# Second-layer rows turned by a crossbar DMA in 16-bit planes, and a reordered token split

## The chip, the cores and the metric

The kernel runs on one core of one Trainium2 chip. The metric is the device time of one execution in microseconds (us), as the median of the runs. An engine name in the rows is short: PE is TensorE, PEld its weight loads, DVE is VectorE, ACT is ScalarE, POOL is GpSimd, and SP is SyncE. SPq and ACTq are the DMA issues of SP and ACT.

## What is computed

Three stages follow each other. The change lies in the third (the second mixture of experts, called second layer here) and in the routing work that is done beside the middle one.

```python
def _moe_ref(x, w_gate, w_val, w_out):            # middle stage: 2304 tokens, 512 -> 1536 -> 512
    g = x @ w_gate
    return (g * (1 / (1 + np.exp(-g))) * (x @ w_val)) @ w_out

def _moe2_ref(x, w_gate, w_output_gate, w1, w2):  # last stage: 8 experts, 512 -> 1024 -> 512
    logits = x @ w_gate
    e_idx = np.argmax(logits, axis=1)
    ...                                           # gate_w: softmax value of the chosen expert
    eom = 1.0 / (1.0 + np.exp(-(x @ w_output_gate)))
    for e in range(E):
        mask = e_idx == e
        h = np.maximum(x[mask] @ w1[e], 0.0)
        out[mask] = gate_w[mask, None] * eom[mask, e, None] * (h @ w2[e])
```

## The kernel before

Every product is made of three float32 matmuls: each operand is split into a high part and a low part (what the high part leaves), and high*high, high*low and low*high are added in PSUM. So each matrix that goes into TensorE is first written twice, by ACT (high) and by DVE (low).

**Middle stage.** The loop over W goes through 4 blocks of 512 tokens; each block has 12 steps c. In a step PE makes the gate product and the value product (24 matmuls) and the output product of the step before (12 matmuls). Beside it, for W of 1 and more, the tokens of block W-1 are routed. On DVE this is `route(c)` (from L997): at c = 1, 2, 5 and 6 it splits a tile of y into three bf16 parts (`y_split_by_token`, L863 to L872, which waits for ACT's first part, `y_high`); at c = 4 and 8 it chooses the expert (`choose`); at c = 5 and 9 it finds each token's place (`place_tokens`) and writes one-hot matrices (`one_hots`, L921 to L925); at c = 6 and 10 it adds the result of PE to `places`. PE multiplies the one-hots in `place` (L1449) at the end of steps 5 and 9. SP turns the three bf16 parts with a DMA transpose (L413).

**Second layer.** The tokens are gathered by expert into tiles of 128 rows. Here there are 20 tiles: tiles 0 and 1 are written out by hand, tiles 2 to 19 run in a loop on each engine. For tile t PE does: `layer1` half 0 (12 matmuls of 512 columns, L1576), 6 matmuls of half 1, `turn_h(t, 0)` (4 transposes of the activations, L1591), the other 6 matmuls of half 1, `turn_rows(t+1)` (4 transposes of the next tile's rows out of `xg`, L1462), 3 matmuls of `layer2` (L1604), `turn_h(t, 1)`, and 21 more of `layer2`. Beside it:

- ACT: `relu(t, 0)` (L739), `h_high(t, 0)` (L734), `rows_high(t+1)` (L717, reads bank 2, into which PE turned the rows), `h_high(t, 1)`, `share(t)`.
- DVE: `h_low(t, 0)` (L1104), the relu of half 1 (L1241, signals `hb_ready`), `rows_low(t+1)` (L1099, signals `xt_ready`), `h_low(t, 1)`, `share(t)`, `scaled(t)` (L1113, needs `scale_in`, frees bank 7 by `o_ready`).
- POOL: waits for `xt_done` of tile t+1, gathers tile t+2 into `xg` by an indirect DMA (L559, L561), waits for the scatter of the tile before (`o_out`), copies the row numbers (L574, L575), looks the scales up by an indirect DMA (L533), and scatters the tile's result (L538) once `scaled(t)` is done.
- `share(t)` is this tile's share, if it has one, of splitting the next expert's weights: 4 chunks by ACT (`e_high`, L703) and DVE (`e_low`, L1095). SP loads the weights in bursts of 8 chunks of 512 KB (L424).

Each engine works through its instructions in the order of the program. Waits of PE in a tile: `ht_ready` (from `h_low(t, 0)`) ahead of layer2, `hb_ready` ahead of `turn_h(t, 1)`, `ht_ready` (from `h_low(t, 1)`) ahead of the 13th matmul of layer2, `o_ready` of the tile before ahead of layer2, and `xt_ready` ahead of layer1. `alone(engine, value)` puts a value into a register for a wait; it costs a register instruction.

Of the kernel before, what the change touches and what calls it, by code (L numbers as in the profile page):

```python
# [16 lines left out]
ALU = mybir.AluOpType  # L17
ACT = mybir.ActivationFunctionType
# [3 lines left out]
BF16 = mybir.dt.bfloat16  # L22
I32 = mybir.dt.int32
U32 = mybir.dt.uint32

P = 128


def build(nc, qT, kT, v, v_tail, w_phi, w_gate, w_val, w_out, w_router, w_outgate, w12, out):
# [4 lines left out]
    DM = H * D  # L34
# [41 lines left out]
    with ExitStack() as ctx:  # L76
        def sb(name, shape, dt=F32, scope=ctx):
            return scope.enter_context(nc.sbuf_tensor(name, shape, dt))
# [98 lines left out]
        h_sb = sb("h_sb", [P, EF])  # L177
        o_sb = sb("o_sb", [P, DM])
        row_in = sb("row_in", [P, 1], U32)
        row_out = sb("row_out", [P, 1], U32)  # L180
        place_rows = sb("place_rows", [P, PLACES], U32)
        scale_at = sb("scale_at", [P, PLACES], U32)
# [8 lines left out]
        t_i, t_per, t_rank, t_from, t_to, t1, t2, t3 = (sb(f"tt{i}", [P, SLOTS]) for i in range(8))  # L191
        n_used, n_tiles = (sb(n, [P, 1]) for n in ("n_used", "n_tiles"))
        eid_f, start_f = (sb(n, [P, E]) for n in ("eid_f", "start_f"))

        bank2 = [ctx.enter_context(nc.psum_tensor(f"bank{i}", [P, 2 * 512], F32)) for i in range(4)]
        bank = [bank2[i // 2][:, i % 2 * 512:(i % 2 + 1) * 512] for i in range(8)]
# [67 lines left out]
        second_in = sem("second_in")  # L264
        sc_in = sem("sc_in")
        xt_done = sem("xt_done")
        xthi_ready = sem("xthi_ready")
        xt_ready = sem("xt_ready")
        l1_done = sem("l1_done")
# [21 lines left out]
            return h_hi[:, c // 2, c % 2] if c < 4 else h_lo[:, c // 2 - 2, c % 2] if c < 8 else h_y[:, c - 8]  # L291

        TURNED = (NW - 1) * WT

        def both(x):

# [157 lines left out]
        def _(pool):  # L454
# [2 lines left out]
            pool.memset(ident[:], 0.0).then_inc(consts, 1)  # L457
            pool.memset(v_sb[:, :, :, D:V1, :], 1.0).then_inc(consts, 1)
            for i, (s, n) in enumerate(((lg_done, 1), (l2_done, 1), (o_ready, 1), (y_crossed, 32),
                         *((s, 16) for s in y_out))):  # L460
                pool.memset(credit[:, i:i + 1], 0.0).then_inc(s, n)
            pool.wait_ge(ones_ready, 1)
# [100 lines left out]

            pool.wait_ge(col_ready, 1)

            def gather_ahead(t):
                pool.wait_ge(xt_done, alone(pool, t + 2))
                gather(t + 2, pool.value_load(table[0:1, bass.ds(t + (T_COL + 2), 1)], min_val=0, max_val=PLACES - 1))

            def tile(t):  # L570
                gather_ahead(t)
                pool.wait_ge(o_out, alone(pool, t * 16))
                col = pool.value_load(table[0:1, bass.ds(t + T_COL, 1)], min_val=0, max_val=PLACES - 1)
                pool.tensor_copy(row_out[:], place_rows[:, bass.ds(col, 1)]).then_inc(ro_ready, 1)  # L574
                pool.tensor_copy(scale_row[:], scale_at[:, bass.ds(col, 1)]).then_inc(sr_ready, 1)  # L575
                pool.wait_ge(ro_ready, alone(pool, t - 1))
                pool.wait_ge(sr_ready, alone(pool, t - 1))
                scale_lookup(scale_rows, NT, scale_row[:, 0:1])
                scatter(t, row_out[:, 0:1])

            gather_ahead(0)
            gather_ahead(1)
            scatter(1, early_rows[:, 1:2])
            pool.wait_ge(tab_ready, 1)
            tiles = pool.value_load(table[0:1, T_TILES:T_TILES + 1], min_val=TILES, max_val=SLOTS)
# [2 lines left out]
            with pool.Fori(2, tiles) as t:  # L588
                tile(t)
            pool.wait_ge(xg_in, alone(pool, tiles * 16 + 16))  # L590
            pool.wait_ge(o_out, alone(pool, tiles * 16))

        @block.scalar
        def _(act):
# [142 lines left out]
            def relu(t, half):  # L737
                act.wait_ge(l1_done, t * 2 + (half + 1))
                act.activation(h_sb[:, half * 512:(half + 1) * 512], bank[half][:], ACT.Relu  # L739
                               ).then_inc(hb_ready if half else ha_ready, 1)  # L740

            def share(t):
                act.wait_ge(tab_ready, 2)
                h0 = act.value_load(table_w[0:1, bass.ds(t + W_FROM, 1)], min_val=0, max_val=2 * (E + 1))
                h1 = act.value_load(table_w[0:1, bass.ds(t + W_TO, 1)], min_val=0, max_val=2 * (E + 1))
                with act.If(h0 < h1):
                    with act.Fori(h0, h1) as half:
                        for i in range(HALF):
                            e_high(half, (half % 4) * HALF + i, i)
# [11 lines left out]
            store_scales(scale_rows, TILES, 2)  # L761
            h_high(1, 1)
            rows_high(2)
            share(1)

            tiles = act.value_load(table[0:1, T_TILES:T_TILES + 1], min_val=1, max_val=SLOTS)
            with act.Fori(2, tiles) as t:
                relu(t, 0)
                h_high(t, 0)
                rows_high(t + 1)  # L770
                h_high(t, 1)
                share(t)

        @block.vector
        def _(dve):
# [215 lines left out]
            def wide(W, first):  # L991
                def low(c):
                    dve.wait_ge(hi_ready, W * FC + (c + 1))
                    dve.tensor_tensor(both(h_lo[:, c % 2]), both(prod[:]), both(h_hi[:, c % 2]), ALU.subtract
                                      ).then_inc(lo_ready, 1)

                def route(c):  # L997
                    V = W - 1
                    for t, step in enumerate((1, 2, 5, 6)):
                        if c == step:  # L1000
                            y_split_by_token(V, t)
                    for i in range(2):
                        g, base = V * 2 + i, V * (2 * STEPS_R) + (i * STEPS_R + STEPS_0)
                        if c == 4 + 4 * i:
                            choose(g, base)
                        if c == 5 + 4 * i:
                            place_tokens(g, base)
                            one_hots(g)
                        if c == 6 + 4 * i:
                            add_places(g)  # L1010

                for c in range(FC):
                    if not first:
                        route(c)
                    dve.wait_ge(silu_done, W * FC + (c + 1))
                    if c or not first:
                        dve.wait_ge(lo_ready, W * FC + c)
                    dve.wait_ge(val_done, W * FC + (c + 1))
                    dve.tensor_tensor(both(prod[:]), both(silu[:]), bank[V_BANK][:], ALU.mult).then_inc(prod_ready, 1)  # L1019
                    low(c)  # L1020
# [196 lines left out]
                                         in1=t3[0:1, :], op0=ALU.min, op1=ALU.add).then_inc(tab_ready, 1)  # L1217


            def share(t):  # L1220
                dve.wait_ge(tab_ready, 2)
                h0 = dve.value_load(table_w[0:1, bass.ds(t + W_FROM, 1)], min_val=0, max_val=2 * (E + 1))
                h1 = dve.value_load(table_w[0:1, bass.ds(t + W_TO, 1)], min_val=0, max_val=2 * (E + 1))
                with dve.If(h0 < h1):
                    with dve.Fori(h0, h1) as half:
                        for i in range(HALF):
                            e_low(half, (half % 4) * HALF + i, i)
# [8 lines left out]

            tiles = dve.value_load(table[0:1, T_TILES:T_TILES + 1], min_val=TILES, max_val=SLOTS)
            with dve.Fori(2, tiles) as t:
                h_low(t, 0)
                dve.wait_ge(l1_done, t * 2 + 2)  # L1240
                dve.tensor_scalar(h_sb[:, 512:1024], bank[1][:], 0.0, None, ALU.max).then_inc(hb_ready, 1)  # L1241
                rows_low(t + 1)
                h_low(t, 1)
                share(t)
                scaled(t)

        @block.tensor
        def _(pe):
# [394 lines left out]
            with pe.Fori(2, tiles) as t:  # L1643
# [4 lines left out]
                layer1(t, rank, 1, 0, 2)  # L1648
                turn_h(t, 0)
                layer1(t, rank, 1, 2, KC)  # L1650
                turn_rows(t + 1)
                layer2(t, rank, 0, 1)
                turn_h(t, 1)
                layer2(t, rank, 1, EC)
# [45 lines left out]
```

## Time and profile before

| what | value |
|---|---|
| median of 3 runs (lowest, highest) | 885.0 us (882.47, 885.52) |
| the profiled execution's own time | 882.82 us |
| its span, first to last instruction | 881.1 us |
| busy share of PE, PEld, DVE, ACT, POOL | 97%, 81%, 44%, 29%, 19% |
| mean granted TensorE clock | 0.995 |
| share of PE in the chain that ended last | 87% |

The profile is one execution. The page lists busy time by engine and by group of instructions; the trace behind it can be asked for a stretch, a line or a tile. A row of a timeline gives start and length in us, the engine, the line of the kernel, the operation with output and inputs, how many were merged, and in brackets how long the engine had been idle before it and what ended that. Matmuls are pipelined, so a matmul of 0.39 us follows the one before after 0.23 us, and a weight load starts together with the matmul before its own.

### The profile page before, as it was taken

The page shows a single profiled execution, that of the slowest core. Times are in us where ns is not written, and L with a number is a line of the kernel's source. Part 1 is how long each engine was busy: PE and PEld are TensorE (multiplying, and loading weights), DVE is VectorE, ACT ScalarE, POOL GpSimd, SP SyncE. Part 2 cuts the span into 40 slices and gives each one's busy share as a digit, 9 for nine tenths or more (in the row PEclk, how much of TensorE's full clock was granted, in tenths as well). Part 3 has the DMA queues.
Part 4 walks back from the last instruction along what each step waited for, and adds up shares of the span by engine and source line. Part 5 has one row for each costly group of instructions (what it writes and reads, how often), then busy time and mean ns, then how long its engine had stood idle before and what let it go on. Part 6 is the DMA issues. An engine that isn't in the chain of part 4 may idle for free.

```text
span 881.1 us, 18909 instructions
## 1 busy us (share of the span) xinstructions
PE 850.6 (97%) x7048; PEld 713.7 (81%) x7049; DVE 385.9 (44%) x770; ACT 257.4 (29%) x387; POOL 163.2 (19%) x222
## 2 busy tenths in 40 slices
PE   8998998999999999999999999999989999999994
PEld 6888897888888788887888788998768888888883
DVE  5776896211132432324323432377774224534431
ACT  4564444111131112211132111325252213323311
POOL 5875300700000000000000000001022233323331
PEclk9999999999999999999999999999999999999997
DMA  9885743500011120203011010106511116116100
GB/s 265 256 240 163 222 139 110 155 0 1 1 61 24 20 65 0 65 18 83 0 48 36 18 42 0 49 2 230 214 49 42 41 48 226 42 39 229 41 25 18
DMA packets 70117, 73.26 MB, mean 83 GB/s; under 512 B 28590, under 2 KB 54830, under 8 KB 70064
## 3 DMA queue, kind: packets, MB, share of 16 engines
q1 hardware_dynamic: 63216, 49.92, 18.8%
q0 software_dynamic: 6560, 22.56, 8.1%
q8 instruction: 40, 0.66, 0.3%
q14 instruction: 13, 0.11, 0.0%
q10 hardware_dynamic: 288, 0.02, 0.0%
HBM read 54.11 MB, written 14.70 MB: 78 GB/s over the span
## 4 chain that ended last, share of the span: by engine, by line
PE 87%; DVE 3%; issue 3%; DMA 3%; ACT 1%; SPq 0%; POOL 0%; POOLq 0%; ACTq 0%; DVEq 0%
PE bank L1381 33%; PE bank L1400 14%; PE bank L1604 11%; PE bank L1576 11%; PE bank L1352 4%; PE bank L1270 4%; PE bank L1297 4%; PE bank L1591 2%; PE bank L1334 1%; PE bank L1462 1%; DMA e_w<-w 1%; PE bank L1371 1%; DMA k_sb<-kT 1%; PE bank L1422 1%; DMA y_rows<-y_sb 1%
## 5 line engine op out<-in xcount | busy, mean ns | idle before, releaser
L1019 DVE TENSOR_TENSOR prod<-silu,bank 128x512 f32<-128x512 f32 x48 | 32.9, 686 | 192.6 <-PE bank L1381 192.6
L1381 PE MATMUL bank<-x_hi,wg_hi 128*128 128x512 f32 (+1 forms) x240 | 90.9, 379 | 0.0
L1381 PE MATMUL bank<-x_hi,wg_lo 128*128 128x512 f32 (+1 forms) x240 | 88.4, 368 | 0.0
L1381 PE MATMUL bank<-x_lo,wg_hi 128*128 128x512 f32 (+1 forms) x240 | 88.3, 368 | 0.0
L1381 PE MATMUL bank<-x_hi,wv_hi 128*128 128x512 f32 (+1 forms) x240 | 88.3, 368 | 0.0
L1381 PE MATMUL bank<-x_lo,wv_hi 128*128 128x512 f32 (+1 forms) x240 | 88.3, 368 | 0.0
L1381 PE MATMUL bank<-x_hi,wv_lo 128*128 128x512 f32 (+1 forms) x240 | 88.3, 368 | 0.0
L528 POOL DMA_INDIRECT stage<-y_rows,early_rows x2 | 2.1, 1066 | 421.5 <-DVE early_rows L977 421.2
L660 ACT ACTIVATE silu<-bank 128x512 f32<-128x512 f32 x48 | 28.7, 598 | 168.3 <-PE bank L1381 168.3
L1400 PE MATMUL bank<-wo_hi,h_hi 128*128 128x512 f32 x192 | 75.5, 393 | 0.0
L1400 PE MATMUL bank<-wo_hi,h_lo 128*128 128x512 f32 x192 | 74.8, 390 | 0.0
L1400 PE MATMUL bank<-wo_lo,h_hi 128*128 128x512 f32 x192 | 74.7, 389 | 0.0
L654 ACT ACTIVATE h_hi<-prod 128x512 fp32r<-128x512 f32 x48 | 30.4, 632 | 150.5 <-DVE prod L1019 150.5
L1604 PE MATMUL bank<-e_hi,hT_hi 128*128 (+1 forms) x160 | 66.3, 414 | 1.5 <-issue 0.9
L1576 PE MATMUL bank<-e_hi,xgT_hi 128*128 (+1 forms) x160 | 64.4, 403 | 0.2 <-DVE xgT_lo L1099 0.2
L1604 PE MATMUL bank<-e_hi,hT_lo 128*128 (+1 forms) x160 | 62.6, 392 | 0.0
L1576 PE MATMUL bank<-e_hi,xgT_lo 128*128 (+1 forms) x160 | 62.6, 391 | 0.0
L1604 PE MATMUL bank<-e_lo,hT_hi 128*128 (+1 forms) x160 | 62.5, 390 | 0.0
L1576 PE MATMUL bank<-e_lo,xgT_hi 128*128 (+1 forms) x160 | 62.3, 390 | 0.0
L1104 DVE TENSOR_TENSOR hT_lo<-bank,hT_hi 128x512 fp32r<-128x512 f32 x40 | 27.7, 692 | 61.6 <-ACT hT_hi L734 60.5
L783 DVE TENSOR_REDUCE amax<-bank 128x8 f32<-128x1024 f32 (+1 forms) x40 | 44.6, 1115 | 20.4 <-PE bank L1270 20.2
L1381 PEld LDWEIGHTS bank<-x_lo,wv_hi 128*128 128x128 f32 x240 | 45.3, 189 | 7.5
(248 smaller groups left out, 1605.3 us busy)
## 6 DMA issues: line engine op xcount, KB each, us to landing
e_w<-w SPq DMA_DIRECT2D x32, 512.0 KB, 5.7
stage<-w_out POOLq DMA_DIRECT2D x16, 384.0 KB, 4.2
y_rows<-y_sb SPq DMA_DIRECT2D x18, 256.0 KB, 2.1
k_sb<-kT SPq DMA_DIRECT2D x16, 256.0 KB, 4.5
v_sb<-v SPq DMA_DIRECT2D x16, 256.0 KB, 4.8
q_sb<-qT SPq DMA_DIRECT2D x16, 256.0 KB, 3.6
x_rows<-x_sb SPq DMA_DIRECT2D x16, 256.0 KB, 3.9
x_in<-x_rows SPq DMA_DIRECT2D x4, 1024.0 KB, 5.7
```

The source lines that it names most:

```text
L654: act.activation(both(h_hi[:, c % 2]), both(prod[:]), ACT.Copy).then_inc(hi_ready, 1)
L660: act.activation(both(silu[:]), bank[G_BANK][:], ACT.Silu).then_inc(silu_done, 1)
L783: dve.tensor_reduce(top, proj, AX.X, ALU.max, apply_absolute_value=True).then_inc(amax_done, 1)
L1019: dve.tensor_tensor(both(prod[:]), both(silu[:]), bank[V_BANK][:], ALU.mult).then_inc(prod_ready, 1)
L1104: dve.tensor_tensor(hT_lo[:, at], bank[6 if half else 3][:], hT_hi[:, at], ALU.subtract).then_inc(ht_ready, 1)
L1270: mm = pe.matmul(acc, src[rows, h, j * P:min((j + 1) * P, S)], phi[rows, :], start=True, stop=True)
L1297: mm = pe.matmul(sums(c, i)[cols, :], feat[:, s, sign, at:at + TAIL], v_sb[:, j, 2 * c + hh, :, a], start=(j == 0 and i in (0, 7)), stop=F ...
L1352: mm = pe.matmul(acc, feat[:, s, sign, half * 512 + i * TAIL:half * 512 + (i + 1) * TAIL], kv_sb[:, b, h // 2 if j < JF else half, sign * ...
L1381: mm = pe.matmul(acc[:, 0:width], w[:, k, cols], x[:, k, 0:width], start=(k == 0 and i == 0), stop=(k == KC - 1 and i == 2))
L1400: mm = pe.matmul(bank[O_BANK + t][:], h[:, c % 2, t // TT, cols], w[:, c, :], start=(c == 0 and i == 0), stop=(c == FC - 1 and i == 2))
L1576: mm = pe.matmul(bank[half][:], x[:, at], w_part(w, rank, k * EF + half * 512), start=(k == 0 and i == 0), stop=(k == KC - 1 and i == 2))
L1604: mm = pe.matmul(bank[7][:], h[:, at], w_part(w, rank, HALF_W + k * DM), start=(k == 0 and i == 0), stop=(k == EC - 1 and i == 2))
```

## The change

Tiles 3 and later of the second layer are no longer turned by PE. The float32 rows are read as pairs of 16-bit words. POOL copies the two words into two planes (`part_words`), ACT issues one DMA transpose of both planes (`cross`), DVE joins the turned planes into `xT` (`merge`), and the high and low parts are made from `xT` in SBUF in place of bank 2 (`merged_high`, `merged_low`). Gathers run three tiles ahead in place of two; tile 3 goes into the second buffer. In the middle stage `y_split_by_token` moves behind `place_tokens`, `one_hots` and `add_places` of the same step.

```diff
             for i, (s, n) in enumerate(((lg_done, 1), (l2_done, 1), (o_ready, 1), (y_crossed, 32),
+                         (x_crossed, 16), (x_merged, 2),
@@ POOL
-            def gather_ahead(t):
-                pool.wait_ge(xt_done, alone(pool, t + 2))
-                gather(t + 2, pool.value_load(table[0:1, bass.ds(t + (T_COL + 2), 1)], min_val=0, max_val=PLACES - 1))
+            def part_words(slot):
+                for half in range(2):
+                    pool.tensor_copy(planes[:, half, :], words(xg_second if slot else xg)[:, :, half]).then_inc(planes_ready, 1)
             def tile(t):
-                gather_ahead(t)
+                pool.wait_ge(xg_in, alone(pool, t * 16 + 16))
+                pool.wait_ge(x_crossed, alone(pool, t * 16))
+                part_words(0)
+                pool.wait_ge(planes_ready, alone(pool, t * 2))
+                gather(t + 3, pool.value_load(table[0:1, bass.ds(t + (T_COL + 3), 1)], min_val=0, max_val=PLACES - 1))
                 pool.wait_ge(o_out, alone(pool, t * 16))
...
-            gather_ahead(0)
-            gather_ahead(1)
+            pool.wait_ge(xt_done, 1)
+            gather(2, column(2))
+            pool.wait_ge(xt_done, 2)
+            pool.tensor_copy(row_second[:], place_rows[:, bass.ds(column(3), 1)]).then_inc(ri_ready, 1)
+            pool.wait_ge(ri_ready, 2)
+            pool.indirect_dma_start(xg_second, None, y_rows, bass.IndirectOffsetOnAxis(ap=row_second[:, 0:1], axis=0),
+                                    bounds_check=NT - 1, oob_is_err=False).then_inc(second_in, 16)
+            pool.wait_ge(xt_done, 3)
+            gather(4, column(4))
+            pool.wait_ge(second_in, 32)
+            part_words(1)
             scatter(1, early_rows[:, 1:2])
@@ ACT
+            def cross(u, n):
+                act.wait_ge(planes_ready, alone(act, n * 2))
+                act.wait_ge(x_merged, alone(act, n * 2))
+                act.wait_ge(consts, 6)
+                act.dma_start_transpose(planesT[:].rearrange("p a (c n) -> p (a c) n", n=P),
+                                        planes[:].rearrange("p a d -> p (a d)")).then_inc(x_crossed, 16)
+            def merged_high(t):
+                act.wait_ge(l1_done, t * 2 + 2)
+                act.wait_ge(x_merged, alone(act, t * 2))
+                act.activation(xgT_hi[:], xT[:], ACT.Copy).then_inc(xthi_ready, 1)
             rows_high(2)
+            cross(3, 1)
             share(1)
             with act.Fori(2, tiles) as t:
                 relu(t, 0)
                 h_high(t, 0)
-                rows_high(t + 1)
+                merged_high(t)
                 h_high(t, 1)
+                cross(t + 2, t)
                 share(t)
@@ DVE
                 def route(c):
-                    for t, step in enumerate((1, 2, 5, 6)):
-                        if c == step:
-                            y_split_by_token(V, t)
                     for i in range(2):
                         ...                       # choose, place_tokens, one_hots, add_places
+                    for t, step in enumerate((1, 2, 5, 6)):
+                        if c == step:
+                            y_split_by_token(V, t)
+            def merge(t):
+                dve.wait_ge(x_crossed, alone(dve, t * 16))
+                for half in range(2):
+                    dve.tensor_copy(words(xT[:])[:, :, half], planesT[:, half, :]).then_inc(x_merged, 1)
+            def merged_low(t):
+                dve.wait_ge(xthi_ready, t + 2)
+                dve.tensor_tensor(xgT_lo[:], xT[:], xgT_hi[:], ALU.subtract).then_inc(xt_ready, 1)
             with dve.Fori(2, tiles) as t:
+                merge(t)
                 h_low(t, 0)
                 ...                               # relu of half 1
-                rows_low(t + 1)
+                merged_low(t)
@@ PE
                 layer1(t, rank, 1, 2, KC)
-                turn_rows(t + 1)
                 layer2(t, rank, 0, 1)
```

## Rows read from the trace of the kernel before

**Rows 1.** Windows: one tile each; busy us by engine (instructions), clock, DMA share, GB/s.

```profile
645.39:659.78 14.39, 13.06 (x61) 10.40 (x62) 9.81 (x13) 9.19 (x12) 4.72 (x7) 1.00 0.19 56
...
728.64:740.92 12.28, 12.28 (x62) 10.19 (x61) 3.52 (x6) 2.39 (x4) 3.59 (x6) 1.00 0.52 161
```

**Rows 2.** Timeline of a tile: start us, us, engine, line, operation, [idle before <-releaser].

```profile
738.63 0.69 DVE L1104 TENSOR_TENSOR hT_lo<-bank,hT_hi 128x512 fp32r<-128x512 f32 x1 [3.85 <-ACT hT_hi L734]
...
738.96 0.39 PE L1576 MATMUL bank<-e_hi,xgT_lo 128*128 x1
...
739.19 0.60 PE L1462 MATMUL bank<-ident,stage 128*128 128x128 f32 x4
739.39 0.69 DVE L1241 TENSOR_SCALAR h_sb<-bank 128x512 f32<-128x512 f32 x1
...
740.09 0.40 PE L1604 MATMUL bank<-e_hi,hT_lo 128*128 x1
740.13 0.55 PEld L1591 LDWEIGHTS bank<-ident,h_sb 128*128 128x128 f32 x4
```

**Rows 3.** Timeline, the last step-5 value and output products and place, W of 1.

```profile
296.99 0.39 PE L1400 MATMUL bank<-wo_hi,h_lo 128*128 128x512 f32 x1
...
297.49 0.35 DVE L925 TENSOR_SCALAR hot_col<-iota_f,g_col,token_no 128x144 fp32r<-128x144 f32 x1
...
298.18 0.44 PE L1381 MATMUL bank<-x_hi,wg_hi 128*128 128x512 f32 x1
```

**Rows 4.** Timeline, the same place in step 9 of the same W.

```profile
331.71 0.40 PE L1400 MATMUL bank<-wo_hi,h_lo 128*128 128x512 f32 x1
...
332.13 0.44 PE L1381 MATMUL bank<-x_hi,wg_hi 128*128 128x512 f32 x1
```

**Rows 5.** Timeline, the engines beside PE from tile 1's end into tile 2.

```profile
645.65 1.05 POOL L561 DMA_INDIRECT stage<-y_rows,row_in  x1 [0.85 <-POOL row_in L559]
646.17 3.90 ACT L703 ACTIVATE e_hi<-e_w  x4 [1.72 <-issue]
...
652.77 0.68 DVE L1104 TENSOR_TENSOR hT_lo<-bank,hT_hi 128x512 fp32r<-128x512 f32 x1
```

**Rows 6.** Tile view of y_tok: durations ns min/median/max, first and last start; time to landing.

```profile
L870 DVE CAST y_tok<-y_sb x12: 427/427/428, 260.4 to 509.4; 128x512 bf16<-128x512 f32 x12
...
L413 SPq DMA_TRANSPOSE y_parts<-y_tok x12: 1280/1430/1543, 261.7 to 513.3; - x12
...
DMA to landing us min/median/max: 3.6/3.7/3.8
```

**Rows 7.** Groups of POOL by line and shape: count, busy us, mean ns, idle before.

```profile
L524 POOL TENSOR_TENSOR wo_lo<-stage,wo_hi 128x768 fp32r<-128x768 f32 x8 | 14.8, 1845 | 48.3 <-DMA x_rows<-x_sb 45.2 <-DMA stage<-w_out 3.0
...
L517 POOL CAST wo_hi<-stage 128x768 fp32r<-128x768 f32 x8 | 6.7, 832 | 4.8 <-DMA stage<-w_out 4.8
...
L559 POOL COPY row_in<-place_rows 128x1 uint32 x20 | 3.7, 186 | 58.3 <-PE bank L1462 56.8 <-issue 1.5
```

**Rows 8.** Timeline, first share tile of the loop and the tile under a weight load.

```profile
656.77 3.91 ACT L703 ACTIVATE e_hi<-e_w  x4 [1.14 <-issue]
...
664.97 0.69 DVE L1104 TENSOR_TENSOR hT_lo<-bank,hT_hi 128x512 fp32r<-128x512 f32 x1 [1.54 <-ACT hT_hi L734]
...
743.96 1.26 POOL L574 COPY row_out<-place_rows 128x1 uint32 x1 [1.17 <-DMA out<-o_sb,row_out]
...
750.91 0.69 DVE L1104 TENSOR_TENSOR hT_lo<-bank,hT_hi 128x512 fp32r<-128x512 f32 x1 [0.49 <-ACT hT_hi L734]
```

**Rows 9.** Timeline, the scales' lookup, PE's last matmul and the scatter of the last tile.

```profile
866.75 1.02 POOL L533 DMA_INDIRECT scale_in<-scale_rows,scale_row  x1 [0.87 <-POOL scale_row L575]
868.10 0.39 PE L1604 MATMUL bank<-e_hi,hT_lo 128*128 x1
868.91 0.75 DVE L1113 TENSOR_SCALAR o_sb<-bank,scale_in 128x512 f32<-128x512 f32 x1 [3.85 <-DMA scale_in<-scale_rows,scale_row]
870.55 1.02 POOL L538 DMA_INDIRECT out<-o_sb,row_out  x1 [2.78 <-DVE o_sb L1113]
```

More of the change, by code:

```diff
@@ L24 @@
 U32 = mybir.dt.uint32
+U16 = mybir.dt.uint16
 P = 128
@@ L179, in build @@
         row_in = sb("row_in", [P, 1], U32)
+        row_second = sb("row_second", [P, 1], U32)
         row_out = sb("row_out", [P, 1], U32)
@@ L193, in build @@
         eid_f, start_f = (sb(n, [P, E]) for n in ("eid_f", "start_f"))
+        planes, planesT = (sb(n, [P, 2, DM], U16) for n in ("planes", "planesT"))
+        xT = sb("xT", [P, KC * P])
         bank2 = [ctx.enter_context(nc.psum_tensor(f"bank{i}", [P, 2 * 512], F32)) for i in range(4)]
@@ L266, in build @@
         xt_done = sem("xt_done")
+        planes_ready = sem("planes_ready")
+        x_crossed = sem("x_crossed")
+        x_merged = sem("x_merged")
         xthi_ready = sem("xthi_ready")
@@ L293, in build, with words @@
         TURNED = (NW - 1) * WT
+        def words(x):
+            return x.bitcast(U16).rearrange("p (n w) -> p n w", w=2)
         def both(x):
@@ L564, in _, with column @@
             pool.wait_ge(col_ready, 1)
-            def gather_ahead(t):
-                pool.wait_ge(xt_done, alone(pool, t + 2))
-                gather(t + 2, pool.value_load(table[0:1, bass.ds(t + (T_COL + 2), 1)], min_val=0, max_val=PLACES - 1))
-            def tile(t):
-                gather_ahead(t)
+            def column(u):
+                return pool.value_load(table[0:1, bass.ds(u + T_COL, 1)], min_val=0, max_val=PLACES - 1)
+            def part_words(slot):
+                for half in range(2):
+                    pool.tensor_copy(planes[:, half, :], words(xg_second if slot else xg)[:, :, half]).then_inc(planes_ready, 1)
+            def tile(t):
+                pool.wait_ge(xg_in, alone(pool, t * 16 + 16))
[3 more added lines that the diff above has]
+                gather(t + 3, pool.value_load(table[0:1, bass.ds(t + (T_COL + 3), 1)], min_val=0, max_val=PLACES - 1))
                 pool.wait_ge(o_out, alone(pool, t * 16))
@@ L590, in _ @@
             pool.wait_ge(xg_in, alone(pool, tiles * 16 + 16))
+            pool.wait_ge(x_crossed, alone(pool, tiles * 16))
             pool.wait_ge(o_out, alone(pool, tiles * 16))
```

## The prediction

> **What bounds the kernel now.** I read the page's part 1 first: PE is busy for 97% of the span, as the table of the section on the profile has it. A busy matmul record overlaps its neighbour, so this share hides short waits. I therefore went on to windows of one tile of the second layer, and then to timelines of the places that the change touches. A tile of the loop takes 12.28 us in which PE shows no gap, while DVE is busy for 3.5 us and ACT for 2.4 us, at a granted clock of 1.00 [rows 1]. Only tile 2, the first of the loop, is longer: 14.39 us. So what counts is PE's order of work, and for each piece taken out of it, what PE must wait for just behind that piece.
>
> **Removed: turn_rows, 18 times.** The reader should look at three starts in [rows 2]. The last matmul of layer1 starts at 738.96 and the third of layer2 at 740.09. That is 1.13 us, and three steps between matmuls are 3 x 0.23 = 0.68 us (738.96 to 739.19 is one step). So turn_rows costs PE 0.45 us, and 18 of them are 8.1 us. Then I ask what is late next. Behind turn_rows come three matmuls and `turn_h(t, 1)`, which needs DVE's relu of half 1. That relu needs the last matmul of layer1 (738.96 + 0.39 = 739.35), starts at 739.39, lasts 0.69 and so ends at 740.08. The weight load of `turn_h(t, 1)` starts at 740.13, where the matmul ahead of it would have let it start at 740.09 [rows 2]. The turn sits exactly at the end of the relu already. Without turn_rows PE would be there at 739.64 and wait until 740.13. The high part is no help either: the first matmul of layer2 needs `h_low(t, 0)`, which runs from 738.63 to 739.32, while PE would now arrive at 739.19. Nothing after the relu becomes shorter. **The period of a plain tile stays at 12.28 us; turn_rows was free.** I put 0 on this term, with 0.04 us on either side for 17 tiles, so -0.7 to +0.7.
>
> **Moved: one-hots ahead of the split.** In step 5 of each W of 1 to 3, DVE splits a tile of y and only then writes the one-hots; the last one-hot starts at 297.49 and PE, whose last output matmul started at 296.99, comes to the next gate product at 298.18 [rows 3]. In step 9, where nothing is split, the same distance is 332.13 - 331.71 = 0.42 us [rows 4]. So the wait costs 1.19 - 0.42 = 0.77 us, three times, 2.3 us. The trace has the same idle time in all three W. With the new order the one-hots start as soon as PE has counted the tokens, before the gate product of the step; the split still waits for ACT's part, as before, so its DMA transpose leaves when it did. **-2.3 us**, and I see nothing that takes its place.
>
> **Added ahead of tile 2: ACT waits for POOL.** `cross(3, 1)` stands ahead of `share(1)` and `relu(2, 0)` on ACT. It needs both planes of tile 3, and POOL makes these only after it issued the gather of tile 4. That issue is the one at 645.65 now, ending at 646.70 [rows 5]. What a plane copy costs on POOL no row shows. The nearest is a cast of 768 elements in 832 ns, so 512 take 0.55 us; the bounds are the 0.19 us of a copy of one element and the two-input operation at 1845 x 512/768 = 1.23 us [rows 7]. I take 0.55, since a copy has one input. The planes are ready at 646.70 + 1.1 + 0.1 = 647.9. The issue of a DMA transpose holds a queue for 1.43 us at 384 KB [rows 6]; for 256 KB I take two thirds, 0.95 us (bounds 0.3 and 1.54). Then `share` needs its register loads and branch, the 1.0 to 1.1 us of idle time marked "issue" [rows 8]. So the weight split starts at about 649.9 in place of 646.17 [rows 5]: 3.7 us later. DVE's four `e_low` follow, then `scaled(1)`, and `h_low(2, 0)` at 652.77 with no idle time before it; PE waits for that one. New on this path are also the two join copies: 0.43 us each by the DVE cast of 512 elements [rows 6], 0.69 as upper bound (`h_low` in [rows 2]), 0.2 as lower. Total 3.7 + 0.9 = **+4.6 us**, once, bounds +2.7 and +7.7. PE has nothing to do meanwhile. The gather of tile 3 goes out ahead of that of tile 4 in time that POOL spent waiting.
>
> **Added to tiles with a share: 5 in the loop.** ACT now issues the crossing between `h_high(t, 1)` and the weight split (+0.95), and DVE joins between `scaled` and `h_low(t+1, 0)` (+0.9). The idle time ahead of that `h_low` is 1.54 us in three such tiles and 0.49 us in the two that run under a weight load, where `scaled` is held by the scales' landing and not by the split [rows 8]. The first kind loses 0.95 + 0.9 - 1.54 = 0.3 us, the second 0.9 - 0.49, with a little for the split, 0.6 us. 3 x 0.3 + 2 x 0.6 = **+2.2 us**, bounds 0 and +5.5.
>
> **Hidden in plain tiles.** The crossing leaves ACT about 4 us before the tile's end, and lands 3.7 us after its issue, by the transposes of y [rows 6]; the join is wanted from DVE 1.3 us after the tile's start, and may be 3 us late before it delays `h_low`. Making `merged_high` and `merged_low` from SBUF is the same count of operations. POOL's new copies fill time in which it waited for `xt_done`.
>
> **The end.** The last `scaled` waits for the scales (866.75 issued, 868.91 used [rows 9]), and PE's last matmul ends at 868.10 + 0.39 = 868.49. POOL no longer waits for turn_rows and issues the lookup 1 to 2 us earlier: **-0.4 us**, bounds -0.5 and 0.
>
> **The sum.** 0 - 2.3 + 4.6 + 2.2 - 0.4 = +4.1 us. On the profiled execution's 882.8 us (span 881.1) this is 886.9. The median is 885.0, 2.2 above it, so I forecast 889.1, rounded to **889.0 us**.
>
> **A rule weighed against the rows.** During a weight split on DVE a POOL copy of one element lasts 1.26 us, as in [rows 8], against the 0.19 of such a copy in [rows 7]. The Trainium skill, "SBUF — State Buffer", section "Who interferes with whom", says why: a DVE instruction with two SBUF inputs and a GpSimd instruction that reads SBUF exclude each other for a whole instruction. The trace agrees. If POOL's plane copies fell into the split of a share tile, the rule would add about 1.1 us to DVE in each of 5 tiles; by POOL's order they come after the scatter, which comes after the split, so my sum goes without it.
>
> **The rivals.**
> (a) PE's gain arrives. If `turn_h(t, 1)` were not bound by the relu, 17 tiles would give 7.7 us: 889.0 - 7.7 = 881.3. Against it stands the start at 740.13 [rows 2], 0.05 us behind the relu.
> (b) The wait ahead of tile 2 is not there, or hidden: 889.0 - 4.6 = 884.4. For it: I infer POOL's and ACT's order from the code, and the issue may be quick. Against it: ACT is in order, and PE waited for the same chain before. With (a) too it would be 876.7.
> (c) Slower: POOL becomes the bound. Its cycle is a closed chain: two plane copies; 0.1; row copy 0.2 after 0.9 of loads; gather 0.85 + 1.05 [rows 5]; two small copies 0.3; lookup 0.87 + 1.02, then 1.14 until `scaled`, then 1.64 until the scatter, 1.02 [rows 9]. Together 9.1 us and the two copies. It decides from (12.28 - 9.1)/2 = 1.6 us a copy. At 1.85 us (the longest POOL operation of [rows 7]) each tile takes 12.8 us, and 17 tiles add about 9 us: 898. A crossing that lands more than 3 us later than those of y, as two do perhaps under a weight load, acts at the same place, DVE's join ahead of `h_low`.
>
> **How the numbers follow.** Forecast 0.50, for 885 to 894 by the bounds of its terms taken together; (b) alone 0.15; (a) alone 0.13; (a) with (b) 0.05; (c) 0.17. About 0.5% (4.4 us) is what a measurement of this kernel can tell from no change. Faster, below 880.6: (a) with (b), and 0.06 of each of (a) and (b), 0.17. Slower, above 889.4: (c) and 0.24 of the forecast, 0.41. Within: 0.42. The range is 880 to 898, which leaves out (a) with (b) and the upper part of (c).
>
> **What would show it.** Plain tiles at 12.28 us with PE idle for about 0.4 us ahead of L1604 or `turn_h(t, 1)`, released by DVE, confirm the first step; 11.8 us refutes it. Tile 2 of about 19 us, with ACT idle ahead of `e_high` until POOL's planes, confirms the third. A plane copy over 1.6 us, or DVE idle ahead of the join for a DMA in plain tiles, means (c). Step 5 without the 0.77 us confirms the second. The prediction is wrong if the join or the plane copies are far from 0.43 and 0.55 us, or if the issue on ACT doesn't hold its queue.

## The result and the profile after

The changed kernel takes 908.15 us (median of 4 runs, 903.62 to 912.19) against 884.24 us before; the ratio is 1.027, interval 1.0215 to 1.0326. That is 24 us slower. I had forecast 889 us and a range up to 898, so the sign was right and the size was not: the time lies outside the range. The profiled execution is the slowest of the four.

The page of the profiled execution (912.19 us, span 910.1), part 1:

```profile
span 910.1 us, 18958 instructions
...
PE 855.8 (94%) x6976; PEld 712.8 (78%) x6977; DVE 399.0 (44%) x806; ACT 257.9 (28%) x387; POOL 184.3 (20%) x264
```

PE has 72 instructions less and a busy share of 94% in place of 97%: it waits more. To see where, I compare the distance between two tiles, from one `turn_h(t, 1)` to the next, read from PE's timeline (the starts of its second group of four transposes in each tile; tile 9, for example, goes from 739.47 to 751.66).

```
us from turn_h(t-1,1) to turn_h(t,1)   t=2    3      4-9    10     11     12-14  15     16     17-19
before                                 16.99  12.27  12.28  12.28  12.28  12.28  12.28  12.28  12.28
changed kernel                         23.44  13.57  12.20  19.06  13.53  12.23  20.49  14.04  12.22
```

The plain tiles are 0.05 to 0.08 us shorter and the time is lost in six tiles: tile 2 (+6.5), tile 3 (+1.3), tiles 10 and 11 (+8.0) and tiles 15 and 16 (+10.0). Together with the plain tiles' -0.8 that is 25 us. The routing of the middle stage gives back 2.3 us. From the place of step 5 (the product with the one-hots) to that of the next block it is 103.13 us before and 102.35 us after, twice, and the first of these places comes 0.71 us sooner after the stage's first gate product. Together this is 22.7 us, which meets the 24 us of the medians within a microsecond or two. In this one execution the span also holds 5.8 us more ahead of the middle stage, in the attention stage, whose code is the same; the first gate product starts anywhere from 147.6 to 156.7 us in the profiled executions of this study, so I count that to none of the parts.

Tile 8's end of the changed kernel, the rows that answer to [rows 2] (a timeline, columns as there):

```profile
737.84 0.69 DVE L1149 TENSOR_TENSOR hT_lo<-bank,hT_hi 128x512 fp32r<-128x512 f32 x1 [3.45 <-ACT hT_hi L764]
...
738.61 0.69 DVE L1297 TENSOR_SCALAR h_sb<-bank 128x512 f32<-128x512 f32 x1
738.67 0.49 PE L1660 MATMUL bank<-e_hi,hT_hi 128*128 x1
...
739.35 0.26 PEld L1647 LDWEIGHTS bank<-ident,h_sb 128*128 128x128 f32 x2 [0.16 <-DVE h_sb L1297]
```

The first matmul of layer2 now comes 0.14 us after `h_low` ended (738.53), and the weight load of `turn_h(t, 1)` 0.05 us after the relu ended (739.30). PE waits twice where the four transposes stood.

The first of the slow tiles, 2, on ACT, DVE and POOL, answering to [rows 5]:

```profile
650.66 1.17 POOL L584 COPY planes<-stage 128x512 uint16<-128x512 uint16 x2
...
652.06 1.35 ACTq L777 DMA_TRANSPOSE planesT<-planes  x1
655.81 3.90 ACT L733 ACTIVATE e_hi<-e_w  x4 [7.41 <-issue]
659.61 0.57 ACT L769 ACTIVATE h_sb<-bank 128x512 f32<-128x512 f32 x1
...
662.40 0.79 DVE L1269 COPY xT<-planesT 128x512 uint16<-128x512 uint16 x2
663.07 0.68 DVE L1149 TENSOR_TENSOR hT_lo<-bank,hT_hi 128x512 fp32r<-128x512 f32 x1
```

ACT sat idle for 7.41 us ahead of `e_high`, first for the planes and then for its own issue, and the relu of tile 2 stands behind the split. PE shows the same as a wait of 6.53 us ahead of `turn_h(2, 0)`; it then runs at a granted clock of 0.50 until 664 us, which stretches the three matmuls ahead of `turn_h(2, 1)` by 0.2 us.

And tile 10, which no term of my sum has. Timeline of the changed kernel again:

```profile
752.45 1.37 ACTq L777 DMA_TRANSPOSE planesT<-planes  x1
...
756.28 1.02 POOL L545 DMA_INDIRECT scale_in<-scale_rows,scale_row  x1 [0.87 <-POOL scale_row L595]
...
767.12 0.75 DVE L1158 TENSOR_SCALAR o_sb<-bank,scale_in 128x512 f32<-128x512 f32 x1 [5.60 <-DMA scale_in<-scale_rows,scale_row]
767.78 0.78 DVE L1269 COPY xT<-planesT 128x512 uint16<-128x512 uint16 x2
768.46 0.68 DVE L1149 TENSOR_TENSOR hT_lo<-bank,hT_hi 128x512 fp32r<-128x512 f32 x1
...
769.28 0.79 PE L1660 MATMUL bank<-e_hi,hT_hi 128*128 x1 [6.32 <-DVE hT_lo L1149]
```

The lookup of 128 scales is issued at 756.28 and used at 767.12; such a lookup lands in 2.6 us at the median. The crossing issued at 752.45 lands after 13.7 us, where the median of all 19 is 3.4. DVE waits 5.60 us for the scales, so `scaled`, the join and `h_low` all come late, and PE waits 6.32 us. The tile view of `planesT` has the spread of the crossings:

```profile
L1269 DVE COPY xT<-planesT x36: 442/450/457, 662.4 to 886.6; 128x512 uint16<-128x512 uint16 x36
L777 ACTq DMA_TRANSPOSE planesT<-planes x19: 1249/1254/1371, 652.1 to 892.9; - x19
...
DMA to landing us min/median/max: 3.1/3.4/14.2
```

What else is in flight is seen in windows of 2 us of both kernels (us, granted clock, DMA share, GB/s). An expert's weights are loaded from 733.98 us before and from 745.39 us after. Before:

```profile
741.00:743.00 2.00, 1.00 1.03 422
743.00:745.00 2.00, 1.00 1.02 414
745.00:747.00 2.00, 1.00 1.00 381
747.00:749.00 2.00, 1.00 0.67 270
749.00:751.00 2.00, 1.00 0.01 0
```

After:

```profile
754.00:756.00 2.00, 1.00 1.02 418
756.00:758.00 2.00, 1.00 1.33 284
758.00:760.00 2.00, 1.00 1.17 119
760.00:762.00 2.00, 1.00 0.97 186
762.00:764.00 2.00, 1.00 0.42 146
764.00:766.00 2.00, 1.00 0.31 112
766.00:768.00 2.00, 0.68 0.01 4
768.00:770.00 2.00, 0.50 0.00 0
```

Before, the load keeps about 400 GB/s until it is done, 15 us after its start. After, the rate is still 418 GB/s in the window ahead of 756 us and 119 from 758 us, some 5 us after the crossing was issued, and the load ends 21 us after its start. The crossing, the lookup and the load's last chunk all land between 766.1 and 767.1 us; the gather issued at 750.98 lands after 9.7 us, where the others take 2.7 to 3.9. The last two windows show a second, small loss: while PE waits, from 763 us on, the granted clock goes to 0.50, the lower of its two levels (1.2 GHz). The stretch from the first matmul of layer2 to `turn_h(10, 1)` then takes 1.54 us (769.28 to 770.82), where tile 8 has 0.80.

### The profile page after: what moved, and what is told of

Read it like the earlier page. It is cut to its first block, busy times and chain, and to the rows that moved or that the text cites. A ratio compares the mean times of both kernels' runs of the same rounds, so it can differ in the third digit from the quotient of the medians.

```text
span 910.1 us, 18958 instructions
## 1 busy us (share of the span) xinstructions
PE 855.8 (94%) x6976; PEld 712.8 (78%) x6977; DVE 399.0 (44%) x806; ACT 257.9 (28%) x387; POOL 184.3 (20%) x264
## 3 DMA queue, kind: packets, MB, share of 16 engines
q10 hardware_dynamic: 20352, 5.00, 3.4%
## 4 chain that ended last, share of the span: by engine, by line
PE 82%; DMA 7%; issue 4%; DVE 3%; ACTq 1%; POOL 1%; ACT 1%; POOLq 0%; SPq 0%; DVEq 0%
PE bank L1437 32%; PE bank L1456 14%; PE bank L1660 10%; PE bank L1632 7%; PE bank L1408 4%; PE bank L1326 4%; PE bank L1353 4%; DMA scale_in<-scale_rows,scale_row 3%; DMA out<-o_sb,row_out 2%; PE bank L1647 1%; PE bank L1390 1%; PE bank L1427 1%; DMA e_w<-w 1%; DMA k_sb<-kT 1%; PE bank L1478 1%
## 5 line engine op out<-in xcount | busy, mean ns | idle before, releaser
L1660 PE MATMUL bank<-e_hi,hT_hi 128*128 (+1 forms) x160 | 68.7, 429 | 17.8 <-DVE hT_lo L1149 16.0
L1660 PEld LDWEIGHTS bank<-e_hi,hT_hi 128*128 128x128 f32 x160 | 31.1, 194 | 31.8 <-issue 25.6
L1437 PEld LDWEIGHTS bank<-x_hi,wg_lo 128*128 128x128 f32 x240 | 45.2, 188 | 7.6
```

The source lines that it names most:

```text
L1437: mm = pe.matmul(acc[:, 0:width], w[:, k, cols], x[:, k, 0:width], start=(k == 0 and i == 0), stop=(k == KC - 1 and i == 2))
L1660: mm = pe.matmul(bank[7][:], h[:, at], w_part(w, rank, HALF_W + k * DM), start=(k == 0 and i == 0), stop=(k == EC - 1 and i == 2))
```

## The experiments

Two theories stood against each other for tiles 10 and 15. A: a crossing and a weight load in flight together slow each other and all that lands then. B: the crossing as such is harmless, and the new order of POOL's work, or the new chain of waits, puts something late. Tile 2 had its own theory, the queue of ACT.

**e1_order: the first part of the change alone, on the kernel before.**

```diff
                 def route(c):
-                    for t, step in enumerate((1, 2, 5, 6)): ...  # y_split_by_token
                     for i in range(2): ...                       # choose, place, one_hots, add_places
+                    for t, step in enumerate((1, 2, 5, 6)): ...  # y_split_by_token
```

> The kernel before with one part of the change alone: in the routing of the middle stage the token split of a step stands behind the one-hots. The theory of the prediction: PE's wait of 0.77 us at the end of step 5 goes in each of three blocks, nothing takes its place, -2.3 us (ratio 0.9974); the distance from the place of step 5 to that of the next block falls from 103.13 to 102.36 us. Rival: the split now stands between the one-hots and the product of its own step, and another wait takes over, ratio 1.000 or above. In the changed kernel the distance is 102.35 us, but its start of the second layer is 4 us later than before, so this run also says whether that shift belongs to this part of the change (then the first gate product, at 149.99 us before and 155.83 us in the changed kernel, comes late here too) or not.

Measured: 879.86 us against 884.16, ratio 0.9958 (0.9937 to 0.9978). From the place of step 5 to that of the next block it is 102.35 us (296.84 to 399.19), as in the changed kernel. In step 5 the last one-hot and PE's use of it stand far apart now:

```profile
291.33 0.35 DVE L925 TENSOR_SCALAR hot_col<-iota_f,g_col,token_no 128x144 fp32r<-128x144 f32 x1
292.79 0.69 DVE L868 TENSOR_TENSOR y_sb<-y_sb,y_tok 128x512 f32<-128x512 f32 x1 [1.11 <-issue]
...
296.61 0.42 PEld L1449 LDWEIGHTS bank<-hot_col,hot_row 128*128 128x128 f32 x2
```

So the part gives 2.3 us by the trace; the ratio says 1.9 to 5.6 us. Its attention stage is not late (first gate product at 149.61), which speaks against this part as the source of the 5.8 us there. All tiles of the second layer take 12.28 us and tile 2 16.98.

**e2_cross_late: the first crossing behind the first weight split.**

```diff
-            cross(3, 1)
             share(1)
+            cross(3, 1)
```

> The changed kernel with one line moved: ACT issues the first crossing behind the first weight split in place of ahead of it. Theory: tile 2 was late because ACT waited for POOL's planes and then for the issue, with the weight split and the relu queued behind. Then the distance from turn_h(1, 1) to turn_h(2, 1), 23.44 us in the changed kernel and 16.99 before, falls to about 18.5 (the relu waits only for the issue of about 1.4 us, and the join for the crossing's landing), some 5 us in all, ratio about 0.022 above before in place of 0.027. Rival: the wait only moves to the join, because the crossing leaves 3 us later than it could, and tile 2 stays above 22 us. Tiles 10, 11, 15 and 16 should stay as late as in the changed kernel by either.

Measured: 900.49 us, ratio 1.018 (1.0139 to 1.0221). Tile 2 takes 17.82 us in place of 23.44, 5.6 us less, and 0.8 more than before. ACT's timeline:

```profile
646.13 2.01 ACT L733 ACTIVATE e_hi<-e_w  x2 [1.78 <-issue]
646.60 1.17 POOL L584 COPY planes<-stage 128x512 uint16<-128x512 uint16 x2
648.00 1.36 ACTq L777 DMA_TRANSPOSE planesT<-planes  x1
648.04 1.99 ACT L733 ACTIVATE e_hi<-e_w  x2
```

The split starts 1.78 us after the row work, as in [rows 5], and ACT's sequencer issues the crossing while its datapath still works off the split. So the loss of tile 2 was the place in ACT's queue. The rival, that the join would wait instead, is out. Tiles 10 and 15 stay at 18.11 and 20.31 us.

**e3_plain_copy: the crossing as a plain copy.** Tiles 3 and later are computed from rows that are not turned.

```diff
-                act.dma_start_transpose(planesT[:].rearrange("p a (c n) -> p (a c) n", n=P),
-                                        planes[:].rearrange("p a d -> p (a d)")).then_inc(x_crossed, 16)
+                act.dma_start(planesT[:].rearrange("p a d -> p (a d)"),
+                              planes[:].rearrange("p a d -> p (a d)")).then_inc(x_crossed, 16)
```

> The changed kernel in which the crossing is a plain DMA of the same 256 KB on the same queue with the same waits; the rows of tiles 3 and later are left unturned, so the result of those tiles is not the reference's. Theory A: the transpose itself, with its many small packets, collapses the DMA rate when it is in flight with a weight load (tiles 10 and 15 of 19.06 and 20.49 us for 12.2). Then a plain copy lands in 3 to 5 us beside the load, those tiles fall to 12.2 to 13.5 us, and the kernel takes about 893 us (ratio 1.010). Theory B: any transfer whose landing DVE needs in that place is as late, and the scales' lookup, which POOL now issues in the midst of the load, is late by itself: then tiles 10 and 15 stay at 19 to 20 us and the ratio at 1.027. The lookup of tile 10 took 10.8 us to land in the changed kernel, 2.4 us in its place before.

Measured: 887.41 us, ratio 1.0039 (1.0014 to 1.0064), less than the 1.010 that theory A had. Tiles 10 and 15 take 12.85 and 12.88 us, tiles 11 and 16 12.69 and 12.72, tile 3 12.23. POOL's order, the waits and the bytes are those of the changed kernel, so theory B falls for this place. The lookups under the load still take 4.9 us to land here, both times, and the gathers 6.3 and 7.2; in the changed kernel it was 10.8 and 12.2, and 9.7 and 8.2. So a load by itself slows them too, but far less. Tile 2 stays at 22.93 us, which agrees with e2: a wait for POOL, not for a landing. Windows of this kernel under a load (busy by engine, then clock, DMA share, GB/s as above), and its issue on ACT from the tile view of `planesT`:

```profile
754.00:756.00 2.00, 2.00 (x10) 1.65 (x9) 1.16 (x2) 2.00 (x3) 0.77 (x3) 1.00 1.04 422
756.00:758.00 2.00, 2.00 (x10) 1.68 (x9) 2.00 (x3) 1.38 (x2) 0.97 (x1) 1.00 1.03 412
```

```profile
L777 ACTq DMA_DIRECT2D planesT<-planes x19: 480/481/537, 652.7 to 875.8; - x19
```

**e7_idle_cross: the crossing by itself, beside the kernel before.** `planes` is set to zero once by POOL; nobody reads `planesT`; the only waits on it are ACT's own, ahead of the next crossing and at the end.

```diff
                 rows_high(t + 1)
                 h_high(t, 1)
+                cross(t)
                 share(t)
```

> The kernel before, with one more DMA transpose of 256 KB of 16-bit zeros per tile, issued by ACT at the place where the change issues its crossing; nothing in the kernel uses it, PE still turns the rows, POOL's order is that of before. This measures the crossing by itself. Theory A (a crossing in flight with a weight load slows both, and all that lands at that time): the crossings of the tiles under a load land after 8 to 14 us in place of 3.4, the scales' lookup and the gather beside them land late, and tiles 10 and 15 take several us more although nobody waits for the crossing: ratio 1.006 to 1.018. Theory B (the order of POOL's work puts the lookup into the load): lookups stay at 2 to 3 us, and only the queue time on ACT shows: the weight split starts 2 us later and share tiles take up to 0.8 us more, ratio 1.000 to 1.004.

Measured: 903.43 us, ratio 1.0221 (1.0184 to 1.0258), more than I had given theory A. Tiles 10 and 15 take 21.32 and 19.89 us, tiles 11 and 16 13.78 and 14.38, tile 2 18.28; tiles without load or split 12.28. Windows of 2 us, and what waited in tile 10:

```profile
744.00:746.00 2.00, 1.00 1.03 418
746.00:748.00 2.00, 1.00 1.36 358
748.00:750.00 2.00, 1.00 1.18 124
750.00:752.00 2.00, 1.00 1.23 101
```

```profile
748.32 1.02 POOL L537 DMA_INDIRECT scale_in<-scale_rows,scale_row  x1 [0.87 <-POOL scale_row L580]
...
761.25 0.75 DVE L1127 TENSOR_SCALAR o_sb<-bank,scale_in 128x512 f32<-128x512 f32 x1 [7.85 <-DMA scale_in<-scale_rows,scale_row]
```

```profile
760.34 1.11 PE L1476 MATMUL bank<-ident,stage 128*128 128x128 f32 x4 [6.18 <-DMA stage<-y_rows,row_in]
```

The crossing was issued at 743.65. No engine is held up by it, yet the lookup that is in flight with it lands after 12.9 us (median 2.3), and PE waits 6.18 us for the rows of the gather issued at 744.45. In the tiles without a load the lookups land in 2.2 to 2.5 us, though a crossing leaves some 3 us ahead of them, so it takes the load too. This run alone shows a loss nearly as large as that of the change, though PE meets it at another wait: for the gathered rows, which the changed kernel fetches a tile earlier.

Tile 2's 1.3 us are not of the crossing, since the first one leaves behind `turn_h(2, 1)` (656.79). The only new work ahead of it is POOL's clearing of `planes` at the end of tile 1, which I take for the cause, though no run leaves it out:

```profile
639.82 0.97 POOL L569 MEMSET planes<- 128x1024 uint16 x1
...
657.59 1.36 ACTq L760 DMA_TRANSPOSE planesT<-planes  x1
```

**e5_split_load: the crossing and the load kept apart in time.** On the changed kernel, SP waits ahead of the fifth of the eight chunks.

```diff
                 for c in range(CH):
+                    if c == HALF:
+                        sp.wait_ge(x_crossed, alone(sp, start * 16 + 16))
                     load_chunk(e, j, c)
```

> The changed kernel with one wait added: SP issues the second four chunks of an expert's weight load only when the crossing of that tile has landed, so a crossing and a load are never in flight together; the bytes, the transposes and POOL's order stay. Theory A (the crossing and the load slow each other when together): every crossing lands in 3 to 4 us, the lookups in 2.3 to 4 us, tiles 10 and 15 (19.06 and 20.49 us in the changed kernel) fall to about 13 us, tiles 11 and 16 stay near 13.5 for the weight split, and some 15 us go: ratio 1.010 (1.005 to 1.014). Theory B (only the wait structure and POOL's order matter): tiles 10 and 15 stay above 17 us. A third way: the second half of the load comes too late for its split and ACT waits for the chunks, then tile 11 and 16 go above 15 us.

Measured: 890.13 us, ratio 1.0078 (1.004 to 1.0115), as theory A had it. Tiles 10, 11, 15 and 16 take 12.88, 13.65, 13.06 and 13.64 us; tile 2 stays at 23.97. The same transposes and the same bytes, one wait more, and 17 us less by the ratios, 13.3 us by the tiles of the loop: theory A. The crossing (745.25) still meets the last of the load's first half, whose traffic ends at 749 us, without such a loss.

**e8_idle_split and e9_idle_split_same_tile: the idle crossing with the load split.**

```diff
+                    if c == HALF:
+                        sp.wait_ge(x_crossed, alone(sp, start * 16 + 32))    # e8; + 16 in e9
```

> The kernel before with the idle crossing of the run e7_idle_cross (which took 1.0221 of the time of before), and the second half of each weight load held until the tile's crossing has landed. Theory A: the idle crossing costs only where it meets the load; kept apart, tiles 10 and 15 fall from 21.32 and 19.89 us to about 12.3 to 13, and what is left is tile 2 (+1.3) and the hold of ACT's queue in tiles with a split (0 to 1 us each): ratio 1.003 (1.000 to 1.007). Theory B (the crossing costs wherever it is issued, for example by what follows it on ACT): the ratio stays above 1.015.

e8 measured 900.82 us, ratio 1.0194 (1.0163 to 1.0225). That was far from the expected 1.003, and the ratio says nothing on the theories, since my count was wrong by one crossing: the second half of a load waited for the next tile's crossing, ACT waited for its chunks, and tiles 11 and 16 took 20.66 and 19.24 us. Tiles 10 and 15, where the crossing now met at most half a load, took 12.50 and 12.27.

> As e8_idle_split, with the count of the wait mended: there the second half of the load waited for the crossing of the next tile, came a tile late, and tiles 11 and 16 took 20.66 and 19.24 us for the chunks. Now it waits for the crossing of its own tile. Theory A (the crossing costs only where it meets the load): tiles 10, 11, 15 and 16 take 12.3 to 13 us, and the ratio is 1.003 (1.000 to 1.007). Theory B (the crossing costs more wherever it is issued): above 1.010.

e9 measured 887.54 us, ratio 1.006 (1.0028 to 1.0092), in place of the 1.0221 of e7. Tiles 10 and 15 take 13.93 and 13.49 us, somewhat more than expected, tiles 11 and 16 12.35 and 12.33, tile 2 18.24. Against e7 this is 14 us by the ratios and 17 us by the tiles: so much the crossing costs where it meets the load. The 4.4 us by which the loop is still longer than before are something else. Tile 2 has the same 1.3 us as in e7, and in tiles 10 and 15 `scaled` waits 1.46 and 1.13 us for the scales, whose lookup meets the second half of the load and lands after 6.5 and 6.2 us:

```profile
753.65 0.75 DVE L1129 TENSOR_SCALAR o_sb<-bank,scale_in 128x512 f32<-128x512 f32 x1 [1.46 <-DMA scale_in<-scale_rows,scale_row]
```

**e6_all and e10_share_first: towards a version without the losses.** e6 joins e2 and e5; e10 also issues the loop's crossing behind the weight split.

```diff
                 h_high(t, 1)
-                cross(t + 2, t)
                 share(t)
+                cross(t + 2, t)
```

> The changed kernel with both cures: the first crossing behind the first weight split, and the weight load in two halves around the crossing. By the terms measured so far against the kernel before: one-hots -2.3 us (ratio 0.9958 as measured alone), plain tiles -0.07 us each or -0.8, tile 2 +0.8, four or five tiles with a split +1.3 each or +5 to +6: about +3 us, ratio 1.003 (0.999 to 1.008). If the crossing has a cost that lies neither in the collision nor in ACT's queue, it is above 1.010. It is not expected to beat the one-hots part alone (0.9958).

e6 measured 888.10 us, ratio 1.0061 (1.0038 to 1.0083).

> The kernel e6_all (ratio 1.0061) with one more line moved: in the loop ACT makes its weight split first and issues the crossing behind it, so the split no longer stands behind the crossing's issue. Theory: tiles with a split (3, 10, 11, 15, 16: 12.9 to 13.65 us in e6_all) lose their 0.7 to 1.4 us because the split starts 2.3 us late behind the crossing; here they come to 12.2 to 12.6 us, about 4.5 us in all, ratio 1.001 (0.998 to 1.004). Rival: the crossing, leaving 5 us later in those tiles, lands after the join should have run, and the same 1 us is lost there (ratio unchanged); by the landing of 3.4 us and the 4.3 us that the join can wait, this should just not happen.

e10 measured 882.33 us, ratio 0.9991 (0.9959 to 1.0024). Tile 3 goes from 13.62 us in e6 to 12.49 and tile 15 from 12.91 to 12.22, as the theory has it; tile 16 hardly moves (13.60 to 13.55), and tile 10 gets worse (12.94 to 14.90). In both, DVE now waits for the scales (2.36 and 3.07 us): POOL's two copies of one element ahead of the lookup run beside the split and last up to 1.2 us each, against 0.2 elsewhere, and the join stands behind `scaled`. With all three cures the loop still takes 5.0 us more than before (230.68 against 225.70 us from `turn_h(1, 1)` to `turn_h(19, 1)`), in an execution of 887.27 us, 5 above its kernel's median; the one-hots give 2.3 back, and the medians show no difference. e1 (0.9958) is the fastest kernel here by the median; its interval and that of e10 overlap.

## Why the prediction was wrong

**turn_rows: right.** I said that removing it gives nothing since the relu of half 1 and `turn_h(t, 1)` come next. The plain tiles went from 12.28 to 12.20 to 12.23 us, 12 of them by 0.07 us on average: -0.8 us, against 8.1 us of removed work. The two waits of PE stand where I put them.

**One-hots: right.** -2.3 us forecast; measured 354.18 us before and 351.90 after from the first gate product to the third place of step 5, -2.3 us, and 0.9958 alone.

**Tile 2: right mechanism, size too small.** Forecast +4.6 us (bounds 2.7 to 7.7), measured 23.44 - 16.99 = +6.5. The plane copies came out at 1.17 us for two (I had 1.1), and the joins put `h_low` 0.67 us later (0.9). The issue on ACT lasted 1.35 us (0.95), and what I had as 1.0 us of register loads behind it took 2.4 us: 652.06 + 1.35 = 653.41, and the split starts at 655.81. The plain copy of e3 has nearly the same 2.2 us behind an issue of only 0.54. A DMA issue doesn't only hold the queue: it looks as if the register loads, which ACT otherwise does while it still computes (1.0 to 1.1 us are left of them in [rows 8]), start after it. No row shows these loads by themselves. The rest is the lower clock, 0.2 us.

**Share tiles: right mechanism, size too small.** Forecast +2.2 us for five (bounds 0 to 5.5). With the collision out of the way (e5), tiles 3, 10, 11, 15 and 16 take 13.56, 12.88, 13.65, 13.06 and 13.64 us, that is +5.4 us. It is the same term: ACT starts the split 2.8 to 3.6 us after `h_high` ended, where it was 1.0 to 1.1, and DVE goes from the split through `scaled` and the join to `h_low` without a pause. e10 takes this away in tiles 3 and 15; in tiles 10 and 16 the scales then hold the same chain.

**The end: nothing.** From `turn_h(19, 1)` to the end of the span it is 18.0 us in both. `scaled` starts 0.67 us after PE's last matmul began, in place of 0.81. The 0.4 us that I had taken are the time from PE's end to DVE's start, of which 0.3 us stay though the scales no longer hold it.

**The step that failed: "a crossing that lands more than 3 us later than those of y, as two do perhaps under a weight load".** I had put this as half a sentence into rival (c), with no price of its own, and priced (c) as a POOL cycle that is too long. That cycle was right (a plane copy takes 0.6 us, so POOL stays well inside 12.2 us) and irrelevant. The crossing under load lands after 14 us, not 4, and it takes the load, the gather and the lookups with it. In the sum this overlap stood at nothing. Tiles 10, 11, 15 and 16 lose 6.2, -0.1, 7.4 and 0.4 us more than in e5, 13.9 us in all. I had taken the landing of 3.7 us from [rows 6] for every tile. But all twelve of those crossings were in flight with light traffic: [rows 6] has 3.6 to 3.8 us for all of them, and a row that never varies says nothing of a case that it doesn't contain.

The sum by the measured terms: -0.8 - 2.3 + 6.5 + 5.4 + 13.9 = +22.7 us, to 24 measured. Without the last term, and with my own sizes for the others, it was +4.1. The bounds of my terms, simply added, reach from 884 to 897 and not only from 885 to 894, and the upper bound of the tile 2 term comes to 7.0 by its rows, not 7.7; neither would have reached 908.

What stays open is where in the DMA path the collision happens. ACT's queue has 20,352 packets for 19 crossings and two small stores, 3,024 with the plain copies of e3, and 288 before: 1,056 packets for a crossing and 144 for a plain copy of the same 256 KB. The DMA share stands above 1 while the rate falls. That it is the number of small packets is an argument; the runs only show that it is the transpose, and that it takes the load beside it.

## What to carry to other kernels

Work taken off the busiest engine gives nothing if the next thing on that engine already starts as its own input lands: look at the start of the next instruction but one and compare it with the end of what it waits for, before counting the removed time. When a transfer is added, ask what is in flight with it in every tile, bursts that come only twice among them, and don't price it by rows from a quiet stretch. And place a DMA issue behind the work of its queue that somebody waits for: it holds back what follows by more than its own length. Last, look at what an experiment adds of its own: 1.3 us of a run that was meant to measure the crossing alone lie ahead of its first crossing.

## What the runs showed of the hardware

A DMA transpose of 256 KB from SBUF to SBUF lands in 3.1 to 4.8 us where no load is in flight (17 of 19; the median of all is 3.4) and in 13.7 and 14.2 us beside a load of 4 MB, and the load's rate falls from about 400 GB/s to between 101 and 186; a plain copy of the same size on the same queue leaves it at 412 to 422 GB/s. The Trainium skill, "DMA: Bandwidth & Descriptors", section "Rules for kernel authors", says that a transpose next to ordinary DMAs needs nothing, which it says of correctness among transposes; for the time, the measurement here decides otherwise, +19 us in e7 for 18 crossings that nobody used, of which 1.3 lie ahead of the first one.

The issue of a transpose keeps ACT's queue for 1.25 to 1.37 us, that of a plain DMA of the same size for 0.48 to 0.54 us.

In a wait of PE of 6.3 us the granted clock fell from 1.00 to 0.50, and it came back only 4 us after the wait's end at 769.28: the window from 768 to 774 us has 0.54, the one before it, with the start of the fall, 0.95 (windows of the changed kernel, columns as in [rows 1]):

```profile
756.00:768.00 12.00, 6.96 (x33) 5.44 (x31) 5.51 (x6) 4.62 (x6) 1.02 (x1) 0.95 0.70 142
768.00:774.00 6.00, 4.72 (x14) 3.87 (x15) 3.10 (x6) 1.23 (x2) 3.46 (x5) 0.54 0.26 72
```

The contention that the prediction left out of its sum is visible and cheap: POOL's two plane copies take 1.17 us in 14 of 19 tiles, and 1.62 to 1.70 us in the five where they meet `merged_low`, which reads twice from SBUF and itself takes up to 1.06 us in place of 0.69. The tile that uses this `merged_low`, 12, still takes 12.23 us.

```profile
783.92 1.65 POOL L584 COPY planes<-stage 128x512 uint16<-128x512 uint16 x2
...
784.04 1.06 DVE L1273 TENSOR_TENSOR xgT_lo<-xT,xgT_hi 128x512 fp32r<-128x512 f32 x1
```
